# A chunked recurrence beside a matmul chain: TensorE takes the carried part and the state directly behind the scores

## The chip, the cores and the metric

The kernel runs on one core of one Trainium2 chip. The metric is the device time of one execution in microseconds; the figure for the kernel before is the median of three runs.

## The reference

```python
for t in range(S):                                   # batch 4, heads 8, S 768, D 40
    m_new = np.maximum(f_gate[:, :, t] + m, i_gate[:, :, t])
    f_stab = np.exp(f_gate[:, :, t] + m - m_new)
    i_stab = np.exp(i_gate[:, :, t] - m_new)
    C = f_stab * C + i_stab * np.einsum('bhd,bhe->bhde', vt, kt)
    n = f_stab * n + i_stab * kt
    h_tilde = np.einsum('bhde,bhe->bhd', C, qt)
    denom = np.maximum(np.abs(np.einsum('bhd,bhd->bh', n, qt)), 1.0)
    y[:, :, t] = sigmoid(o_gate[:, :, t]) * h_tilde / denom
x = y as [3072, 320]
h = x @ w_in                                         # 320 x 2048
x = (max(h, 0) + alpha * min(h, 0)) @ w_out          # 2048 x 320
h = max(x @ w1, x @ w2, x @ w3)                      # 320 x 768 each
return h @ w_out2                                    # 768 x 320
```

## The kernel before

The recurrence is cut into 24 chunks of 128 tokens (six for each of four batches). Within a chunk all eight heads are done at once: scores (k times q, masked by decays), values (scores times v), the carried part (q times the state at the start of the chunk) and the new state. The layer behind it works on blocks of 2, 3, 3, 4, 4, 4, 4 chunks, so on 256, 384 or 512 columns. For each block it runs 16 "hidden" and 16 "project" steps of 8 matmuls each. While TensorE works on block b, the chunks of block b + 1 are woven in. The last layer runs alone at the end, from about 432 us.

The order of work is one list, `EVERY`, made by `first_plan` and `block_plan`. Each engine runs through the same list and does its own part of each step, waiting on semaphores where it needs another engine. For a chunk the steps are ("scores", ch), ("carry", ch), ("values", ch), ("finish", ...), with "gate" and "pack" for ScalarE and "pack" and "prepare" for GpSimd. A hidden or project step lies between the scores and the carry step. In the blocks of four chunks the order is (H hidden, P project):

```
first chunk:   H0 scores H1 [sigmoid] carry H2 values gate P0 gate finish H3 finish pack prepare P1 pack H4
second chunk:  scores P2 carry H5 P3 values gate ...
third chunk:   P5 scores H8 carry P6 values gate H9 ...
fourth chunk:  H11 scores P9 carry H12 values gate P10 ...
```

The block of chunks 8 to 11 has the same order at 384 columns. Chunks 5, 6 and 7 are spread over a whole block of their own, with more hidden and project steps between them.

What each step does on which engine:
- scores: TensorE does 2 x 4 matmuls (line 653, 16 in the trace), VectorE multiplies each half by the decays (line 1059, tile `prob`) and takes its remainder (line 1063), GpSimd the remainder of that (line 1318).
- carry: TensorE does 3 matmuls for the carried part (line 661) and 3 for the state (line 669), 6 each in the trace. VectorE scales the carried part (line 1073) and makes the new state (lines 1082, 1086).
- values: TensorE does 24 matmuls in bf16 (lines 691, 693, 695), and VectorE sums them (line 1102).
- hidden: ScalarE does a relu of the negated bank (line 913, tile `g_full`), VectorE combines (line 1151), ScalarE rounds it (line 922, tile `g_hi`) and VectorE takes the remainder (line 1132, tile `g_lo`); the last two are done one hidden step later. The project step needs `g_lo`.
- sigmoid (line 828) needs another function table on ScalarE than the exponentials of the gate steps (line 886), so a table is loaded before and after it.

Chunk work on TensorE writes to a ring of three PSUM banks. `TASKS` lists the tasks in the order of `EVERY`: scores0, scores1, carry, state, values0, values1 for a chunk, and one for a turn (transposing a finished chunk). A task takes the bank of the task three before it and waits until that one's reader is done (`drained`): for state this is `prob_done` of scores0, which VectorE signals from line 1059. `UNSPLIT` is 5, the first chunk of the third block; from there on the values are done in three bf16 parts.

Of the kernel before, what the change touches and what calls it, by code (L numbers as in the profile page):

```python
# [62 lines left out]
UNSPLIT = FIRST[2]  # L63
# [115 lines left out]
def high(ap):  # L179

    return ap.bitcast(BF16)[(slice(None),) * (len(ap.shape) - 1) + (slice(1, None, 2),)]
# [7 lines left out]
def build(nc, f_g, i_g, q_t, k_t, kv, o_g, w_in, w_out, alpha, w_max, w_out2, out):  # L189
    with ExitStack() as ctx:  # L190
# [371 lines left out]
        def _(pe):  # L562
# [5 lines left out]
            def turns(n):  # L568

                if n == 0:  # L570
                    pe.wait_ge(gates_done, 1)
                    pe.wait_ge(ident_set, 1)
                    span, table_rows, at = SPANS[0], (V,), 0
                if n == 1:
                    pe.wait_ge(exps_done, 1)
                    pe.wait_ge(tables_set, 1)
                    span, table_rows, at = SPANS[0], (E, W), PLAIN * B * H
                if n == 2:
                    pe.wait_ge(exps_done, 2)
                    pe.wait_ge(gated, 1)  # L580
                    span, table_rows, at = SPANS[1], (V, E, W), 0
                for row in table_rows:
                    for c in range(*span):
                        ins = pe.transpose(turned_at[n][:, at:at + B * H], gates[0:B * H, row, c * L:(c + 1) * L],
                                           ident[0:B * H, 0:B * H])
                        at += B * H
                ins.then_inc(turned, 1)

            def bcast(ch):

                if ch == 0:
                    pe.wait_ge(pick_set, 1)
                    pe.wait_ge(later_set, 2)
                    pe.wait_ge(gates_done, 1)
                if ch == 2:
                    pe.wait_ge(gates_done, 2)
                    pe.wait_ge(gated, 3)
                t = slice(ch * L, (ch + 1) * L)
                for g in range(NG):
                    ps = spread[ch][g]  # L600
                    for k in range(HG):
                        pe.matmul(ps[:, k * L:(k + 1) * L], ident_b[:, :], later[:, :], start=(k == 0), stop=False,
                                  skip_group_check=True)
                    for k in range(HG):
                        ins = pe.matmul(ps[:, k * L:(k + 1) * L], pick[:, g * HG + k, :], gates[:, U, t],
                                        start=False, stop=True, skip_group_check=True)
                    ins.then_inc(spread_out, 1)

            def decays():

                pe.wait_ge(last_set, 1)
                pe.wait_ge(tables_set, 3)
                pe.matmul(acc[0][:, 256:256 + NCH * H], last[:, :], tables[:, 1, :, :].rearrange("p c h -> p (c h)"),
                          start=True, stop=True).then_inc(decays_out, 1)
# [14 lines left out]
            def task(part, ch):  # L629

                n = TASKS.index((part, ch))
                if n >= RING_BANKS:
                    pe.wait_ge(*drained(n - RING_BANKS))
                return ring[n % RING_BANKS]

            def attention(step):
                kind, ch = step[0], step[-1]
                if kind == "decays":
                    return decays()
                ch = step[1]  # L640
                if kind == "turns":
                    turns(ch)
                if kind == "bcast":
                    bcast(ch)
                c = ch % SLOTS
                nth = ch // SLOTS + 1
                if kind == "products" or (kind == "scores" and ch >= PLAIN):
                    pe.wait_ge(qk_loaded[c], QK_LOADS * nth)
                    for g in range(NG):
                        ps = task(f"scores{g}", ch)  # L650
                        for k in range(HG):
                            h = g * HG + k
                            ins = pe.matmul(ps[:, k * L:(k + 1) * L], kt[0:KR, c, h % KH * NK + h // KH, :], qt[0:KR, c, h // KH, :],  # L653
                                            start=True, stop=True)
                        ins.then_inc(scored, 1)
                if kind == "carry" and ch:
                    ps = task("carry", ch)
                    pe.wait_ge(state_ready, ch + 1)
                    for g in range(NK):
                        o = g * KH * DE  # L660
                        ins = pe.matmul(ps[:, g * COLS:(g + 1) * COLS], qt[0:KR, c, g, :], state[0:KR, o:o + COLS],  # L661
                                        start=True, stop=True)
                    ins.then_inc(carry_out, 1)
                if (kind == "carry" and ch != 1) or kind == "late":
                    ps = task("state", ch)
                    pe.wait_ge(v_weighted, ch + 1)
                    for g in range(NK):
                        o = g * KH * DE
                        ins = pe.matmul(ps[0:KR, g * COLS:(g + 1) * COLS], nat[:, c, g * KR:(g + 1) * KR],  # L669
                                        v_w[:, c, o:o + COLS], start=True, stop=True)  # L670
                    ins.then_inc(state_out, 1)
                if kind == "values":
                    if ch < UNSPLIT:
                        pe.wait_ge(nat_loaded[c], 16 * nth)
                    else:
                        pe.wait_ge(v_packed, ch - UNSPLIT + 1)
                    for g in range(NG):
                        ps = task(f"values{g}", ch)
                        if ch < UNSPLIT:
                            pe.wait_ge(prob_done, NG * ch + g + 1)  # L680
                            for k in range(HG):
                                h = g * HG + k
                                v = VO + h * DE
                                ins = pe.matmul(ps[:, k * 3 * DE:k * 3 * DE + DE], prob[:, h, :], nat[:, c, v:v + DE],
                                                start=True, stop=True)
                        else:
                            pe.wait_ge(prob_split, NG * (ch - UNSPLIT) + g + 1)
                            for k in range(HG):
                                h, o = g * HG + k, k * 3 * DE
                                v = v_parts[:, h, :, :].rearrange("p n d -> p (n d)")  # L690
                                pe.matmul(ps[:, o:o + 3 * DE], high(prob[:, h, :]), v, start=(k == 0), stop=False,  # L691
                                          skip_group_check=True)
                                pe.matmul(ps[:, o:o + 2 * DE], high(prob_r[:, h, :]), v[:, 0:2 * DE], start=False,
                                          stop=False, skip_group_check=True)
                                ins = pe.matmul(ps[:, o:o + DE], prob_3[:, h, :], v[:, 0:DE], start=False,
                                                stop=True, skip_group_check=True)
                        ins.then_inc(values_out, 1)
                if kind == "turn":
                    ps = task("turn", ch)
                    pe.wait_ge(y_ready, ch + 1)  # L700
                    at = ch - FIRST[BLOCK_OF[ch]]
                    for a in range(3):
                        ins = pe.transpose(ps[:, a * 128:(a + 1) * 128], y[:, at, Y_AT[a]:Y_AT[a] + 128], ident[:, :])
                    ins.then_inc(turned_out, 1)
# [48 lines left out]
            for s in EVERY:  # L753
                layer1(s) if s[0] in LAYER1 else attention(s)
# [624 lines left out]
```

## Time and profile before

| | us |
|---|---|
| median of three runs | 756.58 (755.68 to 757.09) |
| the profiled execution | 756.52 |
| its span | 754.8 |
| TensorE busy in it | 744.0 (99%) |
| VectorE, ScalarE, GpSimd busy | 465.2, 307.1, 184.9 |

The profile is of one execution. PE is TensorE, PEld its weight loads, DVE VectorE, ACT ScalarE, POOL GpSimd, SP SyncE. A line of the timeline has the start of a run of like instructions, the time that it covers, engine, line, operation and tiles; in brackets stands how long the engine had been idle before it and what ended that. Matmuls are pipelined, so each lasts longer than its distance to the next one; distances between starts tell the throughput.

### The profile page before, as it was taken

The page shows a single profiled execution, that of the slowest core. Times are in us where ns is not written, and L with a number is a line of the kernel's source. Part 1 is how long each engine was busy: PE and PEld are TensorE (multiplying, and loading weights), DVE is VectorE, ACT ScalarE, POOL GpSimd, SP SyncE. Part 2 cuts the span into 40 slices and gives each one's busy share as a digit, 9 for nine tenths or more (in the row PEclk, how much of TensorE's full clock was granted, in tenths as well). Part 3 has the DMA queues.
Part 4 walks back from the last instruction along what each step waited for, and adds up shares of the span by engine and source line. Part 5 has one row for each costly group of instructions (what it writes and reads, how often), then busy time and mean ns, then how long its engine had stood idle before and what let it go on. Part 6 is the DMA issues. An engine that isn't in the chain of part 4 may idle for free.

```text
span 754.8 us, 11652 instructions
## 1 busy us (share of the span) xinstructions
PE 744.0 (99%) x4472; PEld 658.5 (87%) x4472; DVE 465.2 (62%) x792; ACT 307.1 (41%) x646; POOL 184.9 (25%) x213
## 2 busy tenths in 40 slices
PE   9889999999999999999999999999999999999998
PEld 6889999999988888888888888888888888888887
DVE  8877788789788758875887646724342423324232
ACT  6655654653564446435643347221212112121211
POOL 6794334355244324432442000000000000000000
PEclk9999999999999999999999999999999999999999
DMA  9963232232232214221300090030201002010100
GB/s 233 289 194 114 79 105 67 85 108 67 80 111 83 75 41 135 70 82 46 101 1 1 21 296 1 0 119 1 78 0 44 34 1 76 1 36 0 36 1 35
DMA packets 30407, 55.66 MB, mean 74 GB/s; under 512 B 3176, under 2 KB 19024, under 8 KB 29968
## 3 DMA queue, kind: packets, MB, share of 16 engines
q1 hardware_dynamic: 29888, 54.49, 23.6%
q8 instruction: 35, 0.57, 0.3%
q10 hardware_dynamic: 464, 0.43, 0.2%
q14 instruction: 20, 0.16, 0.1%
HBM read 46.96 MB, written 7.95 MB: 73 GB/s over the span
## 4 chain that ended last, share of the span: by engine, by line
PE 87%; DVE 3%; POOL 3%; issue 2%; DMA 2%; SPq 1%; ACT 0%; POOLq 0%; DVEq 0%; ACTq 0%
PE bank L767 26%; PE bank L730 21%; PE bank L745 5%; PE bank L747 5%; PE bank L746 5%; PE bank L653 4%; PE bank L782 3%; PE bank L784 3%; PE bank L783 3%; PE bank L749 3%; PE bank L750 3%; PE bank L669 2%; PE bank L661 2%; DMA u_bcast<-u_scratch 2%; PE bank L691 1%
## 5 line engine op out<-in xcount | busy, mean ns | idle before, releaser
L730 PE MATMUL bank<-x_split,w_hi 128*128 128x512 f32 (+2 forms) x560 | 168.2, 368 | 0.0
L730 PE MATMUL bank<-x_split,w_lo 128*128 128x512 f32 (+2 forms) x336 | 120.9, 362 | 0.0
L913 ACT ACTIVATE g_full<-bank 128x512 f32<-128x512 f32 (+2 forms) x112 | 59.8, 534 | 140.6 <-PE bank L730 139.6
L730 PEld LDWEIGHTS bank<-x_split,w_hi 128*128 128x128 f32 x560 | 103.3, 190 | 12.3 <-ACT x_split L871 0.3
L1151 DVE SCALAR_TENSOR_TENSOR g_full<-g_full,beta,bank 128x512 f32<-128x512 f32 (+2 forms) x112 | 74.7, 667 | 40.4 <-ACT g_full L913 39.8
L1132 DVE TENSOR_TENSOR g_lo<-g_full,g_hi 128x512 fp32r<-128x512 f32 (+2 forms) x112 | 77.8, 694 | 28.6 <-ACT g_hi L922 27.9
L1172 DVE TENSOR_TENSOR best<-bank,first_of_max 128x512 f32<-128x512 f32 x36 | 24.9, 692 | 102.4 <-PE bank L767 76.1
L745 PE MATMUL bank<-g_hi,wproj 128*128 128x512 f32 (+2 forms) x224 | 84.5, 377 | 3.2 <-DVE g_lo L1132 3.2
L922 ACT ACTIVATE g_hi<-g_full 128x512 fp32r<-128x512 f32 (+2 forms) x112 | 63.1, 563 | 51.1 <-DVE g_full L1151 50.9
L747 PE MATMUL bank<-g_hi,wproj 128*128 128x512 f32 (+2 forms) x224 | 80.9, 361 | 0.0
L746 PE MATMUL bank<-g_lo,wproj 128*128 128x512 f32 (+2 forms) x224 | 80.6, 360 | 0.0
L954 ACT ACTIVATE g_hi<-best 128x512 fp32r<-128x512 f32 x36 | 22.8, 632 | 128.7 <-DVE best L1176 128.7
L767 PE MATMUL bank<-x_split_b,w_hi 128*128 128x512 f32 x270 | 70.4, 391 | 0.0
L767 PE MATMUL bank<-x_split_a,w_hi 128*128 128x512 f32 x270 | 70.4, 391 | 0.0
L730 PEld LDWEIGHTS bank<-x_split,w_lo 128*128 128x128 f32 x336 | 64.2, 191 | 6.8
L1318 POOL TENSOR_TENSOR prob<-prob_rest 128x512 bf16<-128x512 f32 x38 | 42.8, 1126 | 75.2 <-DVE prob_rest L1063 75.2
L767 PEld LDWEIGHTS bank<-x_split_a,w_hi 128*128 128x128 f32 x270 | 50.1, 188 | 9.5
L767 PEld LDWEIGHTS bank<-x_split_b,w_hi 128*128 128x128 f32 x270 | 50.0, 188 | 9.3
L886 ACT ACTIVATE u_bcast<-u_bcast,tables 128x128 f32<-128x128 f32 x168 | 52.4, 390 | 0.1
L1307 POOL TENSOR_TENSOR v_rest<-kv,v_parts 128x320 f32<-128x320 f32 x19 | 15.1, 797 | 140.7 <-ACT v_parts L862 140.7
L745 PEld LDWEIGHTS bank<-g_hi,wproj 128*128 128x128 f32 x224 | 42.5, 190 | 8.1 <-DVE g_lo L1132 3.8
L1176 DVE TENSOR_TENSOR best<-bank,best 128x512 f32<-128x512 f32 x36 | 24.9, 692 | 39.5 <-PE bank L767 39.5
(135 smaller groups left out, 1453.3 us busy)
## 6 DMA issues: line engine op xcount, KB each, us to landing
u_bcast<-u_scratch SPq DMA_DIRECT2D x21, 512.0 KB, 4.2
kv<-in_kv SPq DMA_DIRECT2D x24, 324.0 KB, 3.0
q_t<-in_q_t SPq DMA_DIRECT2D x24, 180.0 KB
k_t<-in_k_t SPq DMA_DIRECT2D x72, 60.0 KB
out<-final SPq DMA_DIRECT2D x5, 640.0 KB, 3.8
wproj_raw<-in_w_out SPq DMA_DIRECT2D x4, 640.0 KB, 10.5
o_gate<-in_o_gate SPq DMA_DIRECT2D x4, 640.0 KB, 4.9
w_raw<-in_w_max SPq DMA_DIRECT2D x2, 1152.0 KB, 6.7
```

The lines of the kernel that those rows point to most:

```text
L653: ins = pe.matmul(ps[:, k * L:(k + 1) * L], kt[0:KR, c, h % KH * NK + h // KH, :], qt[0:KR, c, h // KH, :], start=True, stop=True)
L730: ins = pe.matmul(ps[:, 0:cols], w[:, a, f], xs[:, x, 0:cols], start=(m == 0), stop=(m == 7))
L745: pe.matmul(acc[a][:, 0:cols], wa, hi, start=(j == 0), stop=False)
L746: pe.matmul(acc[a][:, 0:cols], wa, lo, start=False, stop=False)
L747: pe.matmul(acc[a][:, 0:cols], wl, hi, start=False, stop=(j == J1 - 1))
L767: ins = pe.matmul(ps[:, :], w[:, a, cols], x2[b2 % 2][:, x, :], start=(k == 0), stop=(k == 7))
L886: ins = act.activation(ub[:, c, h, :], src, ACT.Exp, bias=tables[:, 0, ch, h:h + 1])
L913: act.activation(gf[:, n % GF_SLOTS, 0:cols], hid[j % HID_BANKS][:, 0:cols], ACT.Relu, scale=-1.0).then_inc(neg_done, 1)
L922: act.activation(gh[:, n % G_SLOTS, 0:cols], gf[:, n % GF_SLOTS, 0:cols], ACT.Copy).then_inc(g_hi_done, 1)
L1132: dve.tensor_tensor(gl[:, n % G_SLOTS, 0:cols], gf[:, n % GF_SLOTS, 0:cols], gh[:, n % G_SLOTS, 0:cols].bitcast(F32), ALU.subtract).then_i ...
L1151: dve.scalar_tensor_tensor(out=g, in0=g, scalar=beta[:, j:j + 1], in1=hid[j % HID_BANKS][:, 0:cols], op0=ALU.mult, op1=ALU.add).then_inc(h ...
L1318: pool.tensor_tensor(prob_3[:, heads, :], prob_r[:, heads, :], high(prob_r[:, heads, :]), ALU.subtract).then_inc(prob_split, 1)
```

## The change

For chunks 5 to 23, TensorE issues the matmuls of the carried part and of the state as part of the scores step, directly behind those of the scores, and nothing in the carry step. The list of tasks, the banks and the order of work on all other engines stay as they are. Chunks 0 to 4 are unchanged.

```diff
-                if kind == "carry" and ch:
+                joined = ch >= UNSPLIT
+                if (kind == "carry" and ch and not joined) or (kind == "scores" and joined):
                     ps = task("carry", ch)
                     pe.wait_ge(state_ready, ch + 1)
                     for g in range(NK):
...
                     ins.then_inc(carry_out, 1)
-                if (kind == "carry" and ch != 1) or kind == "late":
+                if (kind == "carry" and ch != 1 and not joined) or kind == "late" or (kind == "scores" and joined):
                     ps = task("state", ch)
                     pe.wait_ge(v_weighted, ch + 1)
                     for g in range(NK):
```

## Rows read from the trace of the kernel before

**Rows 1.** The page, part 1: busy us, share of the span, instructions.
```profile
PE 744.0 (99%) x4472; PEld 658.5 (87%) x4472; DVE 465.2 (62%) x792; ACT 307.1 (41%) x646; POOL 184.9 (25%) x213
```
**Rows 2.** Waits of TensorE: who waited for whom, us in total, times, longest.
```profile
PE bank L745 <- DVE g_lo L1132: 3.2, 3, 2.5
PE bank L703 <- DVE y L1118: 2.5, 1, 2.5
```
**Rows 3.** Timeline of TensorE, chunk 12.
```profile
205.54 1.95 PE L653 MATMUL bank<-q_t,k_t 120*128 120x128 f32 x16
207.25 0.48 PE L730 MATMUL bank<-x_split,w_hi 128*128 128x512 f32 x1
207.57 0.40 PE L730 MATMUL bank<-x_split,w_lo 128*128 128x512 f32 x1
...
209.17 0.83 PE L661 MATMUL bank<-state,q_t 120*128 120x128 f32 x6
209.84 0.83 PE L669 MATMUL bank<-v_weighted,kv 128*120 128x128 f32 x6
210.42 0.47 PE L730 MATMUL bank<-x_split,w_hi 128*128 128x512 f32 x1
```
**Rows 4.** Timeline of TensorE, the scores of chunks 5, 9, 10 and 13.
```profile
84.25 1.95 PE L653 MATMUL bank<-q_t,k_t 120*128 120x128 f32 x16
...
154.83 1.95 PE L653 MATMUL bank<-q_t,k_t 120*128 120x128 f32 x16
...
168.73 1.95 PE L653 MATMUL bank<-q_t,k_t 120*128 120x128 f32 x16
...
220.68 1.95 PE L653 MATMUL bank<-q_t,k_t 120*128 120x128 f32 x16
```
**Rows 5.** Timeline of VectorE, first product of chunks 5, 9, 10, 12 and 13.
```profile
85.50 0.69 DVE L1059 TENSOR_TENSOR prob<-bank,u_bcast 128x512 f32<-128x512 f32 x1
...
157.46 0.68 DVE L1059 TENSOR_TENSOR prob<-bank,u_bcast 128x512 f32<-128x512 f32 x1
...
170.76 0.68 DVE L1059 TENSOR_TENSOR prob<-bank,u_bcast 128x512 f32<-128x512 f32 x1
...
207.04 0.69 DVE L1059 TENSOR_TENSOR prob<-bank,u_bcast 128x512 f32<-128x512 f32 x1
...
220.61 0.78 DVE L1132 TENSOR_TENSOR g_lo<-g_full,g_hi 128x512 fp32r<-128x512 f32 x1 [0.71 <-ACT g_hi L922]
221.51 0.75 DVE L1151 SCALAR_TENSOR_TENSOR g_full<-g_full,beta,bank 128x512 f32<-128x512 f32 x1
222.18 0.69 DVE L1059 TENSOR_TENSOR prob<-bank,u_bcast 128x512 f32<-128x512 f32 x1
```
**Rows 6.** Timeline of ScalarE, one row ahead of chunk 9, then chunk 12 to 13.
```profile
156.12 0.47 ACT L913 ACTIVATE g_full<-bank 128x384 f32<-128x384 f32 x1
...
209.37 0.60 ACT L913 ACTIVATE g_full<-bank 128x512 f32<-128x512 f32 x1 [1.58 <-PE bank L730]
209.98 1.28 ACT L828 ACT_TABLE_LOAD   x1
...
219.59 0.48 ACT L865 ACTIVATE v_parts<-v_rest 128x320 bf16<-128x320 f32 x1 [0.89 <-POOL v_rest L1307]
...
220.88 0.60 ACT L913 ACTIVATE g_full<-bank 128x512 f32<-128x512 f32 x1 [0.30 <-PE bank L730]
```
**Rows 7.** Waits of all engines: a weight load of the values for the carried part.
```profile
PEld bank L691 <- DVE carried L1073: 0.2, 1, 0.2
```
**Rows 8.** Stretches: length, busy us by engine (instructions), TensorE's granted clock, DMA share, GB/s.
```profile
26.00:29.40 3.40, 0.94 (x9) 0.93 (x9) 2.96 (x8) 3.37 (x7) 0.79 (x2) 1.00 1.08 249
29.40:32.90 3.50, 3.50 (x18) 3.24 (x17) 2.62 (x5) 1.96 (x5) 3.44 (x5) 0.51 1.06 302
39.70:43.10 3.40, 1.39 (x12) 1.18 (x11) 1.32 (x2) 1.23 (x4) 3.40 (x5) 1.00 1.09 269
43.10:46.50 3.40, 2.87 (x13) 2.87 (x14) 3.36 (x8) 2.50 (x8) 2.97 (x5) 0.50 0.97 297
```

## The prediction

> **What bounds the kernel now.** I read the busy times first: TensorE works 744.0 us of a span of 754.8 [rows 1]. Next came the list of waits of its engine. It has five entries, all before the sixth chunk's work; the two largest are in [rows 2]. So in the region of the change (84 to 432 us, blocks 1 to 5) TensorE never idles by the profile. It sets the end, and every new wait there adds to the time unless something that it issues gets shorter. After that I read the timeline around single chunks, engine by engine, to see how late each engine could be without TensorE noticing.
>
> **What is moved.** For 19 chunks (5 to 23) the six matmuls of the carried part (C) and the six of the state (T) come directly behind the 16 of the scores (S), and the hidden or project step that stood between comes after them. Nothing is removed or added; no DMA is moved in its queue. The operands of C and T are ready early: the state vector since the chunk before, the weighted v since two chunks before. The loads of q and k that wait for T can start about 1.5 to 1.9 us sooner; SP had no late load in this region and none of its transfers appears among TensorE's waits, so I cost that at nothing, in both directions.
>
> **What the switches of kind cost.** In chunk 12, S starts at 205.54, the first matmul of the next hidden step at 207.25, its second at 207.57, C at 209.17, T at 209.84, hidden again at 210.42 [rows 3]. A matmul of C or T stands 0.11 us behind the last (0.67/6). The first big matmul behind small ones takes 0.32 us to its successor instead of 0.23. That looks like 0.09 us per return to big matmuls, and the move takes away one return per chunk. But 16 matmuls at 0.1115 should take 1.78 us and S took 1.71: the last small one is followed 0.07 us early. Net, one return costs 0.02 us. Gain: 19 x 0.02 = **-0.4 us**. The other end is the face value, 19 x 0.085 = -1.6 us.
>
> **The new wait.** The PSUM ring has three banks, and tasks take them in turn: scores0, scores1, carry, state. So T writes the bank of scores0 and must wait until VectorE has multiplied it (`prob_done`, line 1059). Before, a big step (1.4 to 1.9 us) lay between; now only scores1 and C do. T's first weight load would go out 21 spacings behind the first of S: 21 x 0.1115 = S + 2.34 us. Behind a waiting T stand the project or hidden steps, so the whole wait is lost. When is VectorE done? I set its first `prob` of a chunk against the start of that chunk's scores:
> - chunk 5: 84.25 against 85.50 + 0.69, ready at S + 1.94 [rows 4, 5]. Chunks 7, 8 and 11 are the same within 0.05, chunk 6 is at 1.78: no wait, 0.35 us or more spare.
> - chunk 12: 205.54 [rows 3] against 207.04 + 0.69: ready at S + 2.18. With some 0.05 for the signal this is 0.1 us ahead of 2.34: no wait, but hardly any cover. Chunks 15, 16, 19, 20, 23 are alike; 14, 18 and 22 are at 1.79.
> - chunk 9: 154.83 against 157.46 + 0.68: S + 3.31, a wait of 1.0 us already by these rows. Chunk 10: 168.73 against 170.76 + 0.68: S + 2.70, a wait of 0.4 us.
> - chunks 13, 17, 21: 220.68 against 222.18 + 0.69: S + 2.18 as well, by the trace of before. But these move.
>
> **What the move itself makes later.** The first chunk of blocks 3 to 5 and chunk 8 have the order hidden0, S, hidden1, C, T, hidden2, values. The move puts hidden1 behind C and T, 12 x 0.1115 = 1.34 us later (the step after it ends where it did before, since only the order inside changed). ScalarE waits for just that step: its relu at 209.37 had been idle 1.58 us for TensorE [rows 6]. Behind that relu stand two table loads of 1.28 us, the sigmoid of a whole block and eight exponentials, back to back, and none of it can start before: no idle entry stands between 209.37 and the 0.89 us at 219.59, and that one is a wait for GpSimd, whose step follows ScalarE's own one before it. Only at 220.88 does ScalarE wait for TensorE again, and only 0.30 us. So the 1.34 us of delay travels the whole way, and at least 1.04 of it arrive at the relu of hidden4.
> - chunk 13: ScalarE's g_hi comes ahead of that relu and ends the full 1.34 later, so VectorE's g_lo, which waited for it, goes from 220.61 to 221.95, and the step behind it to about 222.60, 0.65 us behind (it was at 221.51); the product goes from 222.18 to 223.27 and is done at 223.95, S + 3.27 [rows 5]. With 0.05 for the signal the wait is 3.32 - 2.34 = **0.98 us**. Chunks 17 and 21 have the same rows: 3 x 0.98 = 2.9 us.
> - chunk 9: ScalarE's relu at 156.12 starts with no idle time before it, 1.1 us after its hidden step ended [rows 6], so ScalarE is already the late one and the delay arrives whole: 3.31 + 1.34 = 4.65, wait 4.70 - 2.34 = **2.36 us**.
> - chunk 5 also has this order, but four hidden and project steps more lie before the next scores, and chunk 6's product was waiting for TensorE: covered.
> - chunk 10: its VectorE chain starts anew from a wait for TensorE (behind its hidden6), so it moves with TensorE: wait 2.75 - 2.34 = **0.41 us**. In return the 0.2 us that the values of chunk 10 waited for the carried part [rows 7] go, since VectorE does not move and TensorE comes later: -0.2 us.
> - The third chunks (14, 18, 22 and 10) also have their hidden step moved behind C and T. There VectorE's carried part would end near S + 6.9 and the second half of the values needs it at S + 7.2, and the delay is used up in ScalarE's and VectorE's waits for TensorE before the next scores. In the second and fourth chunks a project step is moved, for which no engine waits.
>
> **The sum.** 2.36 + 0.41 + 2.9 - 0.2 - 0.4 = +5.1 us. The profiled execution took 756.52 us (span 754.8), 0.06 below the median of the runs, so both give the same: **761.6 us**, 0.7% slower.
>
> **The rivals.**
> *The clock falls too.* TensorE was granted its full clock but for two stretches: 29.4 to 32.9 at 0.51 and 43.1 to 46.5 at 0.50, that is the lower of its levels (1.2 instead of 2.4 GHz). Ahead of each it had been busy only 0.94 of 3.40 us and 1.39 of 3.40 us [rows 8], in waits of 2.5 us each [rows 2]. The wait at chunk 9 would be of that size. If the clock falls there for as long, at most half of 3.4 us is lost; I take 1.5: **763.1 us**. Against it: 2.36 is a little shorter, and the matmuls around it are denser. The Trainium skill ("TensorE: Matmul & The Clock Gate", section "Why this matters for your kernels") wants gaps between bursts kept short to avoid throughput drops mid-kernel, and its figure for a harmful gap lies above all waits here; by it there is no fall at chunk 9, while the trace shows one behind each wait of 2.5 us. The measurement decides, so the chance stays with the trace: 0.25.
> *Only block 2 is late.* In the 512-column blocks a step of TensorE is 1.82 us and ScalarE's chain may catch up (GpSimd's part may overlap more than I let it). Then the 2.9 us go: 758.7 us. Against: the back-to-back rows [rows 6]. Chance 0.10.
> *Not slower.* The other side: the delay of ScalarE's chain is absorbed in every block, because the relu of hidden1 is done early enough in slack that I don't see, and only the 1.0 and 0.4 us of chunks 9 and 10 stay. With the returns at face value: 756.5 + 1.4 - 0.2 - 1.6 = 756.1; with my price 757.3. It decides between 0.5 and 1.3 us of slack on ScalarE between the relu of hidden1 and the next scores. The trace has 0.30 in chunk 13, none in chunk 9. Chance 0.13, of which 0.04 for faster.
> *More waits.* The six chunks with 0.1 us of cover miss it, or GpSimd and VectorE slow each other as they meet anew (the remainder at 1063 took 0.69 to 1.5 us in different chunks). Six times 0.3 on top: 763.4 us. Chance 0.10.
>
> **How the numbers follow.** Forecast 0.42, clock 0.25, block 2 alone 0.10, not slower 0.13, more waits 0.10. The range 757.5 to 764.5 leaves out the not-slower case and the joint case of clock and more waits. A measurement can tell about 0.2% (1.5 us) from no change. Slower by more than that (over 758.1): 0.85; within: 0.11; faster: 0.04.
>
> **What would show it.** TensorE's list of waits gets line 669 for VectorE's line 1059: about 2.4 us at chunk 9, 1.0 at chunks 13, 17, 21, 0.4 at chunk 10. If 13, 17 and 21 are missing, the chain through ScalarE was judged wrong; if the small ones (12, 15, 16 ...) appear, the cover of 0.1 us. A granted clock of 0.5 behind chunk 9 shows the clock rival. ScalarE's relu of the step behind C and T should start 1.3 us later against S. The forecast is wrong if T isn't held at all, or if TensorE's small matmuls run closer than 0.11 us when 28 of them stand together.

## The result and the profile after

| | before | after |
|---|---|---|
| median, us | 756.59 (755.68 to 757.09, 4 runs) | 762.75 (761.66 to 763.40, 4 runs) |
| ratio | | 1.0083, 95% interval 1.0067 to 1.0099 |
| profiled execution, its span, us | 756.52, 754.8 | 761.66, 759.9 |

The kernel got 0.8% slower, 6.2 us by the medians. 761.6 had been forecast, in a range of 757.5 to 764.5.

The two profiled executions differ by less (5.1 us). The part ahead of the change varies: the scores of chunk 5, with the same code ahead of them, started at 84.25 us before and at 82.77 us here, and at 83.1 to 85.3 us in the profiles of the experiments below. That 761.66 meets the forecast of 761.6 almost to the digit is therefore luck: the medians stand 1.1 us higher, and so do the terms, as the stretch shows. I therefore compare the traces over one stretch, from the start of the first matmul of the scores of chunk 5 to the start of the last matmul of all. The two ends in the trace of after (timeline of TensorE):

```profile
82.77 1.95 PE L653 MATMUL bank<-q_t,k_t 120*128 120x128 f32 x16
...
756.58 0.31 PE L785 MATMUL bank<-wout_hi,g_lo 128*128 128x320 f32 x1
```
and the last matmul in the trace of before, whose first end is in [rows 4]:
```profile
751.47 0.31 PE L784 MATMUL bank<-wout_hi,g_lo 128*128 128x320 f32 x1
```
That is 673.81 against 667.22 us: **+6.59 us** in the stretch.

TensorE's waits in the changed kernel (engine, tile and line, waited for whom: us in total, times, longest; line 670 is line 669 of before, 1060 is 1059):
```profile
PE bank L670 <- DVE prob L1060: 4.4, 4, 2.1
PE bank L704 <- DVE y L1119: 2.5, 1, 2.5
PE bank L746 <- DVE g_lo L1133: 2.2, 2, 1.7
...
PEld bank L670 <- DVE prob L1060: 5.5, 5, 2.3
```
The first line has taken the top over [rows 2]: the state's matmuls wait for the product that frees the bank of scores0. TensorE as a whole sees four such waits, its weight loads five; the fifth is chunk 10's, of 0.3 us. Below, S + x means x us behind the start of that chunk's scores, and C and T stand for the carried part (line 662) and the state (line 670). Here are chunk 9, with the longest, then chunks 12 (none) and 13, on TensorE:
```profile
153.21 1.95 PE L653 MATMUL bank<-q_t,k_t 120*128 120x128 f32 x16
155.00 0.83 PE L662 MATMUL bank<-state,q_t 120*128 120x128 f32 x6
157.96 1.63 PE L670 MATMUL bank<-v_weighted,kv 128*120 128x128 f32 x6 [2.13 <-DVE prob L1060]
159.25 0.67 PE L746 MATMUL bank<-g_hi,wproj 128*128 128x384 f32 x1
159.71 0.52 PE L747 MATMUL bank<-g_lo,wproj 128*128 128x384 f32 x1
...
207.87 1.95 PE L653 MATMUL bank<-q_t,k_t 120*128 120x128 f32 x16
209.65 0.83 PE L662 MATMUL bank<-state,q_t 120*128 120x128 f32 x6
210.32 0.82 PE L670 MATMUL bank<-v_weighted,kv 128*120 128x128 f32 x6
210.90 0.47 PE L731 MATMUL bank<-x_split,w_hi 128*128 128x512 f32 x1
...
222.98 1.95 PE L653 MATMUL bank<-q_t,k_t 120*128 120x128 f32 x16
224.76 0.83 PE L662 MATMUL bank<-state,q_t 120*128 120x128 f32 x6
226.36 0.92 PE L670 MATMUL bank<-v_weighted,kv 128*120 128x128 f32 x6 [0.76 <-DVE prob L1060]
227.03 0.47 PE L746 MATMUL bank<-g_hi,wproj 128*128 128x512 f32 x1
```
From C to T is 0.67 us where nothing waits (chunk 12). In chunk 13 it is 1.60, so 0.93 us were waited, and T then takes 0.67 instead of 0.58 us to what follows: a wait costs 0.1 us more to start again. In chunk 9 it is 2.96 us: a wait of 2.29 us.

Where the lateness of chunk 13 comes from shows on ScalarE; these lines answer to [rows 6]:
```profile
213.02 0.60 ACT L914 ACTIVATE g_full<-bank 128x512 f32<-128x512 f32 x1 [2.92 <-PE bank L731]
213.64 1.28 ACT L829 ACT_TABLE_LOAD   x1
214.93 1.27 ACT L829 ACTIVATE o_gate<-o_gate 128x1280 f32<-128x1280 f32 x1
...
217.23 1.28 ACT L887 ACT_TABLE_LOAD   x1
218.52 2.45 ACT L887 ACTIVATE u_bcast<-u_bcast,tables 128x128 f32<-128x128 f32 x8
...
223.24 0.48 ACT L866 ACTIVATE v_parts<-v_rest 128x320 bf16<-128x320 f32 x1 [0.89 <-POOL v_rest L1308]
223.61 0.61 ACT L923 ACTIVATE g_hi<-g_full 128x512 fp32r<-128x512 f32 x1
224.13 0.58 ACT L914 ACTIVATE g_full<-bank 128x512 f32<-128x512 f32 x1
```
The first relu now waits 2.92 instead of 1.58 us, 1.34 us more; its hidden step starts 3.03 instead of 1.71 us behind the scores, 1.32 later. Against the scores of chunk 12 it starts at 5.15 instead of 3.83. The last relu no longer waits for TensorE at all: ScalarE has become the late one. On VectorE this gives, ahead of chunk 13 (answering to [rows 5]):
```profile
224.26 0.78 DVE L1133 TENSOR_TENSOR g_lo<-g_full,g_hi 128x512 fp32r<-128x512 f32 x1 [0.71 <-ACT g_hi L923]
224.97 0.73 DVE L1152 SCALAR_TENSOR_TENSOR g_full<-g_full,beta,bank 128x512 f32<-128x512 f32 x1
225.62 0.68 DVE L1060 TENSOR_TENSOR prob<-bank,u_bcast 128x512 f32<-128x512 f32 x1
```
The product is done at 226.30, 3.32 us behind the start of the scores (before: 2.18).

Then there is the clock. The stretches around the wait of chunk 9 (length, busy us by engine, granted clock, DMA; they answer to [rows 8]):
```profile
154.50:157.80 3.30, 1.33 (x12) 1.14 (x11) 2.70 (x5) 1.72 (x4) 3.30 (x4) 1.00 0.00 0
157.80:161.20 3.40, 3.24 (x12) 3.24 (x13) 3.33 (x6) 0.06 (x1) 2.77 (x4) 0.50 0.13 38
```
TensorE was busy 1.33 of 3.30 us, and then was granted 0.50 of its clock, the level of 1.2 GHz, for 3.4 us. Before, the clock was full here. T at chunk 9 took 1.29 us instead of 0.67 to what follows it, and the project step 2.37 instead of 1.48: 1.5 us together.

The +6.59 us of the stretch thus fall into: waits with restart 2.39 (chunk 9), 0.39 (chunk 10), 3 x 1.02 (13, 17, 21) = 5.84; the lower clock 1.5; less 0.23 for the values of chunk 10, which no longer wait for the carried part [rows 7]; less about 0.5 for 19 returns to big matmuls. That makes 6.6.

### The profile page after: what moved, and what is told of

It reads as the page before. It is cut to its first block, busy times and chain, and to the rows that moved or that the text cites. A ratio compares the mean times of both kernels' runs of the same rounds, so it can differ in the third digit from the quotient of the medians.

```text
span 759.9 us, 11652 instructions
## 1 busy us (share of the span) xinstructions
PE 745.5 (98%) x4472; PEld 659.7 (87%) x4472; DVE 466.2 (61%) x792; ACT 306.3 (40%) x646; POOL 185.4 (24%) x213
## 4 chain that ended last, share of the span: by engine, by line
PE 80%; issue 7%; DVE 5%; POOL 3%; ACT 1%; ACTq 0%; POOLq 0%; DVEq 0%
PE bank L768 26%; PE bank L731 18%; PE bank L746 5%; PE bank L748 5%; PE bank L747 5%; PE bank L783 3%; PE bank L785 3%; PE bank L784 3%; PE bank L653 3%; PE bank L750 2%; PE bank L751 2%; PE bank L670 2%; DVE prob L1060 1%; PE bank L662 1%; PE bank L692 1%
```

## The experiments

Each has a median with the ratio to the kernel before on the same chip, and the time of the stretch (chunk 5's scores to the last matmul) in its profiled execution, where before took 667.22 and the changed kernel 673.81 us. Each stretch is that of a single execution; the changed kernel's, taken twice, came out 0.13 us apart. All start from the changed kernel.

**Only the carried part is moved.**
```diff
-                if (kind == "carry" and ch != 1 and not joined) or kind == "late" or (kind == "scores" and joined):
+                if (kind == "carry" and ch != 1) or kind == "late":
```


> Only the carried part is moved behind the scores; the state stays where it was before. If the loss is the state's wait for the bank of scores0, there is none here, since a whole step lies again before the state: 756.6 us, same as before, though the first product of chunk 13 should still come later than before, by about half of what it does in the changed kernel (S + 2.6 to 2.8 instead of S + 3.3), for the hidden step is put off by 0.67 us. If the loss comes from putting off the hidden steps as such (ScalarE and VectorE late for their own work, the wait only a sign of it), half of the loss stays: 759 to 760 us.

756.57 us, ratio 1.0008 (0.9999 to 1.0016); stretch 667.47. The loss is gone with the state's early place, while the product of chunk 13 was later than before by a little under half of what it is in the changed kernel (S + 2.63, against 2.19 before and 3.32). One small thing I had not expected: chunk 9's product came at S + 4.00, so late that even a state behind the project step was held for 0.2 us, and 0.1 more to start again. So putting the hidden steps off by 0.67 us costs nothing where nobody waits; the whole delay of 1.34 us is in the next run and in that of chunks 8, 12, 16 and 20 alone.

**The five late chunks are left out.**
```diff
-                joined = ch >= UNSPLIT
+                joined = ch >= UNSPLIT and ch not in (9, 10, 13, 17, 21)
```


> The change for 14 chunks; chunks 9, 10, 13, 17 and 21 keep the order of before. My theory: all of the loss sits in the state's wait of these five, so no wait of line 669's matmuls is left, and 756.6 - 14 x 0.02 = 756.3 us. If the small covers of 0.1 us (chunks 12, 15, 16, 19, 20, 23) fail or the moved hidden steps hurt elsewhere: 757.5 to 760 us.

756.96 us, ratio 1.0012 (1.0003 to 1.0020); stretch 667.90. Half a miss. Chunks 10, 13, 17, 21 and the six with 0.1 us of cover did not wait, but chunk 9 did, in the order of before:
```profile
154.46 1.95 PE L653 MATMUL bank<-q_t,k_t 120*128 120x128 f32 x16
...
157.66 0.83 PE L662 MATMUL bank<-state,q_t 120*128 120x128 f32 x6
159.21 0.92 PE L670 MATMUL bank<-v_weighted,kv 128*120 128x128 f32 x6 [0.71 <-DVE prob L1060]
```
Chunk 8 still put off its hidden step, so the product of chunk 9 stood at S + 4.69, and the state reached its place at S + 3.87: I had taken the project step for enough cover without setting it against 4.7. At 13, 17 and 21 the products were as late as in the changed kernel (S + 3.32), and nobody waited. The rest checks the price of a return. The stretch grew by 0.68 us: 0.97 for this wait and its restart, and 0.08 that the values of chunk 9 now waited for the carried part, less 14 returns. So one return is 0.026 us.

**The first chunks are left out.**
```diff
-                joined = ch >= UNSPLIT
+                joined = ch >= UNSPLIT and ch not in (8, 12, 16, 20)
```


> The change for all but the first chunks of the blocks (8, 12, 16 and 20 keep the order of before). My theory: the lateness at chunks 13, 17, 21 and 1.3 us of that at chunk 9 come from the hidden step put off one chunk earlier. So chunks 13, 17, 21 do not wait, chunk 9 waits 1.0 us and chunk 10 0.4 us, each 0.1 more to start again: 756.6 + 1.1 + 0.5 - 0.2 - 0.3 = 757.7 us. Rival: the second chunks are late by themselves, because TensorE takes the state too early there: all five waits stay, 761.5 to 762.5 us.

756.86 us, ratio 1.0011 (1.0002 to 1.0020); stretch 668.01. In the trace it is what my theory said: no wait at 13, 17 and 21, 0.90 us at chunk 9 and 0.30 at chunk 10 and 0.1 more each.
```profile
154.96 1.95 PE L653 MATMUL bank<-q_t,k_t 120*128 120x128 f32 x16
156.74 0.83 PE L662 MATMUL bank<-state,q_t 120*128 120x128 f32 x6
158.31 0.92 PE L670 MATMUL bank<-v_weighted,kv 128*120 128x128 f32 x6 [0.74 <-DVE prob L1060]
```
So the second chunks are not late by themselves; leaving four *other* chunks alone took their waits away. The stretch grew by 0.79 (expected: 1.1), since I had counted the waits at chunks 9 and 10 0.1 us too long each and the returns 0.1 too low together; the median grew by 0.5.

**The sigmoid goes to the end of an earlier block.**
```diff
-        if n == 1 and b:
-            both.append(("sigmoid", b + 1))
...
+    if b + 2 < NBLK:
+        both.append(("sigmoid", b + 2))
     return both + [("rows_out", b)]
```


> The whole change, and the sigmoid of a block is done at the end of the block two before it, behind its last turn, where ScalarE was idle for 2.2 to 3.5 us, instead of behind hidden1. Chunk 8 and the first chunks keep the moved hidden step. My theory: what carries the delay is ScalarE's unbroken chain of two table loads, sigmoid and exponentials; without 3.8 us of it ScalarE waits for TensorE again before the next scores, chunks 9, 13, 17 and 21 do not wait, chunk 10 still waits 0.5 us: 756.6 + 0.5 - 0.2 - 0.4 = 756.5 us. Rival: the delay reaches the next scores by VectorE's own queue whatever ScalarE does: 761 to 762.5 us.

756.88 us, ratio 1.0011 (1.0002 to 1.0020); stretch 667.50. The whole change is in, and the hidden step is put off as in the changed kernel, but there was no wait at chunks 13, 17 and 21. ScalarE and VectorE ahead of chunk 13:
```profile
211.00 0.60 ACT L914 ACTIVATE g_full<-bank 128x512 f32<-128x512 f32 x1 [2.91 <-PE bank L731]
...
221.16 0.60 ACT L914 ACTIVATE g_full<-bank 128x512 f32<-128x512 f32 x1 [0.61 <-PE bank L731]
```
```profile
221.79 0.75 DVE L1152 SCALAR_TENSOR_TENSOR g_full<-g_full,beta,bank 128x512 f32<-128x512 f32 x1 [0.42 <-ACT g_full L914]
222.46 0.68 DVE L1060 TENSOR_TENSOR prob<-bank,u_bcast 128x512 f32<-128x512 f32 x1
```
The first relu is put off as in the changed kernel (2.91 us idle), but the last one waits for TensorE again. What carried the delay was ScalarE's chain. The move took less out of it than the 3.8 us that I had expected: one table load of 1.28 us and the sigmoid of 1.27 are gone, but a load still stands ahead of the exponentials, which start 3.85 us behind the first relu (at 214.85) instead of 5.50. That is 1.65 us less, and it accounts for the wait of the last relu: 0.30 before [rows 6], + 1.65 - 1.34 = 0.61, as measured. Chunk 9 was a partial miss: the product came at S + 2.91, a wait of 0.51 us. There ScalarE's last relu (at 155.35) still didn't wait for TensorE, so even the shorter chain is not caught up in time.

No run has the early sigmoid without the rest. But the terms above (0.61 and 0.40 for the waits at 9 and 10 with their restarts, less 0.23 for the values of chunk 10 and 0.49 for 19 returns) give +0.29 us against +0.28 measured, which leaves next to nothing for the move of the sigmoid itself.

**The parts of the change by chunks.** The changed kernel once more, then chunks 12 to 23 alone, 5 to 11 alone, and 8, 12, 16, 20 alone:
```diff
-                joined = ch >= UNSPLIT
+                joined = ch >= 12
```
```diff
-                joined = ch >= UNSPLIT
+                joined = UNSPLIT <= ch < 12
```
```diff
-                joined = ch >= UNSPLIT
+                joined = ch in (8, 12, 16, 20)
```


> The changed kernel once more, for its clock. Its waits at chunks 9, 10, 13, 17 and 21 must come back at 2.3, 0.3, 0.9, 0.9 and 0.9 us. Theory of the clock: a wait of TensorE of 2.3 us brings the lower clock behind it, as at chunk 9 in the first profile; then the profile shows it again, and from the scores of chunk 5 to the last matmul it takes 673.8 us. Rival: the fall there was chance (how the wait lay in time), and a profile without it takes 672.3 us for the same stretch. Median of the runs 762 to 763 us.

> The change for chunks 12 to 23 alone: waits of 0.9 us at 13, 17 and 21 (0.1 more each to start again) and 12 returns less at 0.025 us, no wait in chunks 5 to 11, no fall of the clock there. If the parts add up: 756.5 + 3.05 - 0.3 = 759.2 us, and 2.75 us more than before from the scores of chunk 5 to the last matmul. If the 512-column blocks take some of the wait back: under 758.5 us.

> The change for chunks 5 to 11 alone. Waits at chunks 9 and 10 (2.4 and 0.4 us with starting again), less 0.2 us for the values of chunk 10 and 7 returns at 0.025 us: +2.4 us from the scores of chunk 5 to the last matmul, and +3.9 us where the clock falls behind chunk 9. So 758.9 us without the fall, 760.4 with it.

> The change for chunks 8, 12, 16 and 20 alone, that is only those that put off a hidden step ahead of ScalarE's long chain. The first product of chunks 9, 13, 17 and 21 is as late as in the changed kernel (S + 4.7 and S + 3.3), but their state comes a project step later: only chunk 9 waits, 0.9 + 0.1 us. 756.5 + 1.0 - 0.1 = 757.4 us. Rival: if the delay itself costs, whoever waits for it, near half of the loss is here: 759 us or more.

| | median, us | ratio to before | stretch, against before |
|---|---|---|---|
| the whole change | 762.49 | 1.0088 (1.0076 to 1.0101) | 673.94, +6.72 |
| chunks 12 to 23 | 758.29 | 1.0034 (1.0023 to 1.0046) | 670.02, +2.80 |
| chunks 5 to 11 | 760.11 | 1.0054 (1.0041 to 1.0067) | 671.11, +3.89 |
| chunks 8, 12, 16, 20 | 757.20 | 1.0017 (1.0008 to 1.0026) | 668.20, +0.98 |

The parts add up: 2.80 + 3.89 = 6.69 against 6.59 and 6.72. For 12 to 23 the waits were the expected 0.93 us three times. The median rose by 2.1 us rather than 2.75 and so fell under the 758.5 that I had named for a wait partly taken back. The trace doesn't bear that out: the three waits are whole and the stretch grew by 2.80. The difference is no larger than the part ahead of chunk 5 varies, and 2.75 us lies within the interval of the ratio. For 5 to 11 stretch and median came as expected with the fall of the clock (+3.9, 760.4). The last kernel has the products of chunks 13, 17 and 21 at S + 3.3, as late as in the changed one, and no wait there, only 0.89 us at chunk 9. Again the delay costs nothing where nobody waits for it.

The clock was low behind the wait at chunk 9 in each of the three profiles that have the wait of 2.3 us with nothing in it. Here the two new ones, the whole change and then chunks 5 to 11:
```profile
157.70:161.00 3.30, 1.18 (x10) 0.99 (x10) 2.66 (x5) 1.72 (x4) 3.30 (x4) 1.00 0.00 0
161.00:164.40 3.40, 3.40 (x14) 3.40 (x13) 3.33 (x6) 0.00 (x0) 2.77 (x3) 0.51 0.30 94
```
```profile
155.50:158.90 3.40, 1.42 (x13) 1.23 (x11) 2.80 (x5) 1.74 (x4) 3.40 (x4) 1.00 0.00 0
158.90:162.30 3.40, 3.26 (x12) 3.26 (x13) 3.33 (x6) 0.04 (x1) 2.77 (x4) 0.50 0.15 33
```
In the profiles with 0.9 us of wait at chunk 9, or at 13, 17 and 21, it stayed full. The granted clock of all the runs agrees: its mean over a run was 0.991 to 0.996 in all 14 runs with that wait, but 0.997 or 0.998 in 25 of the 66 runs of the kernel before that were made with the experiments. One fall of 3.4 us is worth 0.002 of that mean.

**The wait is filled.**
```diff
                     ins.then_inc(carry_out, 1)
+                    if ch == 9:
+                        pe.wait_ge(hid_read, 2 * J1 + 5 - HID_BANKS + 1)
+                        for n in range(10):
+                            pe.matmul(hid[1][:, 0:3 * L], w1h[:, 0, 640:768], xs[:, 0, 0:3 * L], start=True, stop=True)
```


> The whole change, and at chunk 9 TensorE does ten useless matmuls of 384 columns between the carried part and the state; they write to the bank that the next hidden step starts afresh. They take 10 x 0.17 = 1.7 us of a wait of 2.3 us, so the state comes no later. Theory: behind the wait at chunk 9 the clock is halved for 3.4 us and that costs 1.5 us by itself; with TensorE busy in the wait there is no fall, and from the scores of chunk 5 to the last matmul it takes 673.8 - 1.5 = 672.3 us, the median is 1.5 us below that of the changed kernel: 761.0 us. Rival: the lower clock costs nothing that the wait doesn't cost already: 762.5 us as before.

761.31 us, ratio 1.0062 (1.0049 to 1.0075); stretch 672.42, 1.4 to 1.5 us less than the two profiles of the changed kernel. TensorE at chunk 9 (lines 668, 674 and 1064 are the filling, the state and the product here), and the stretches around:
```profile
155.95 0.83 PE L662 MATMUL bank<-state,q_t 120*128 120x128 f32 x6
156.54 2.01 PE L668 MATMUL bank<-x_split,w_hi 128*128 128x384 f32 x10
158.91 0.92 PE L674 MATMUL bank<-v_weighted,kv 128*120 128x128 f32 x6 [0.35 <-DVE prob L1064]
```
```profile
154.00:157.40 3.40, 3.40 (x29) 3.40 (x29) 2.26 (x4) 2.43 (x7) 2.15 (x3) 1.00 0.00 0
157.40:160.80 3.40, 3.05 (x20) 2.73 (x19) 3.33 (x6) 0.52 (x1) 3.40 (x4) 1.00 0.00 0
```
The state starts 2.96 us behind the carried part as without the filling, so the product's lateness is untouched; what is gone is the low clock. It cost 1.5 us on its own. With more work the kernel took less time (ratio to before 1.0062 instead of 1.0088; the two intervals don't meet), and the clock's mean was 0.998 in four of its six runs.

**Both: the sigmoid early, and chunks 9 and 10 left out.** The edit is that of the sigmoid above and `joined = ch >= UNSPLIT and ch not in (9, 10)`.

> The sigmoid at the end of an earlier block, and the change for all chunks but 9 and 10, the only two whose state still waited there. No wait for the bank of scores0 is left, 17 returns less at 0.025 us: 0.4 us below the kernel before from the scores of chunk 5 to the last matmul (666.8 us against 667.2), so 756.0 us and no difference that five rounds can tell. If moving the sigmoid costs at the block's end (rows copied later): 757 us.

755.98 us, ratio 0.9995 (0.9986 to 1.0004); stretch 666.78, no wait of the state left. 17 returns less gave 0.44 us in the stretch, 0.026 us each if the early sigmoid costs nothing; as a time it is no difference.

## Why the prediction was right

The sum's terms against what the runs showed, in us:

| term | forecast | measured |
|---|---|---|
| wait at chunk 9 (product done at S + 4.65) | 2.36 | 2.29 (S + 4.69), and 0.1 to start again |
| wait at chunk 10 | 0.41 | 0.29, and 0.1 |
| waits at 13, 17, 21 (S + 3.27) | 0.98 each | 0.93 each (S + 3.32), and 0.1 |
| chunks with 0.1 us of cover | none | none |
| values of chunk 10 | -0.2 | -0.23 |
| 19 returns | -0.4 | -0.5 (0.026 each) |
| starting again after five waits | none | +0.5, as above |
| the clock behind chunk 9 | none (a rival with 1.5) | 1.5, in three profiles of three |
| the stretch | +5.1 | +6.59 and +6.72 |

- *The mechanism* held: the state waits for the bank of scores0, and two causes make it wait. At chunks 9 and 10 VectorE was already late. At 13, 17, 21, and for 1.3 us more at 9, the delay is made a chunk earlier, by putting hidden1 behind C and T, and ScalarE carries it. Taking away either end of that relay (the first chunks' move, or the sigmoid with one of its two table loads) took the waits away at 13, 17 and 21.
- *The sum* is 1.5 us short, all of it the clock. The other errors cancel: 0.5 us for starting again has no term, while the five waits were together counted 0.34 us too long and the gains (values and returns) 0.13 us too small. That the rest fits so well is in part luck.
- *Return to big matmuls:* netting the long first spacing against the short last one was right. At its face value of 0.085 us, 19 returns would have paid 1.6; the two runs that tell it best, with the five late chunks left out and with both remedies, give 0.026 each.
- *The clock* is the step that failed, as a matter of likelihood. I called 2.36 us "a little shorter" than the waits that had brought the clock down and gave the fall 0.25; it came each time, and the likeliest case should have been 763.1, not 761.6. In the prediction's own terms: the chance of the clock rival was set too low. The medians of 762.75 and 762.49 lie 1.1 and 0.9 above the forecast. The trace of before pointed that way: busy 0.94 and 1.39 of 3.40 us ahead of its two falls [rows 8], and the wait at chunk 9 leaves 1.2 to 1.4. It would not have made the fall certain. Ahead of chunk 5 the twelve profiles have 16 waits of 2.2 us or more, and 14 had a fall around or behind them. The other two, of 2.45 and 2.48 us, had none: with the five late chunks left out and with the sigmoid early, TensorE was busy 0.95 and 0.92 of the 3.40 us up to 30.0, and the clock stayed full up to 36.0. And the length of the wait alone doesn't decide: of two waits at the same place, one of 1.51 us (the last run) was followed by a fall and one of 1.48 (chunks 12 to 23) was not. What else decides is open. The Trainium skill ("TensorE: Matmul & The Clock Gate", section "Why this matters for your kernels") wants no gaps over about 3 us and would have let waits of this size pass; these traces don't agree.
- *Only block 2 is late* fell with chunks 12 to 23 alone (+2.80 us). *Not slower* fell too: ScalarE's slack was 0.30 us in chunk 13 as read. *More waits*: the six chunks at S + 2.18 stayed without a wait in every kernel.
- One reading was wrong without a consequence: of TensorE's five waits in the kernel before, four lie ahead of chunk 5, but the fifth (0.4 us, line 782) stands at 749.76 in the last layer, behind the region of the change.
- What stays open is why the part ahead of chunk 5 varies by some 2 us from run to run with the same code. It is larger than several effects here; no run was made for it. The traces show where it sits: TensorE's wait for `g_lo` that ends near 43 us (line 746) lasted 1.70 us in the first profile of the changed kernel and 3.62 in the second, which reached chunk 5 at 82.77 and 85.30. And it goes with the clock: of the 66 runs of the kernel before, the 14 with a mean granted clock of 0.993, the lowest among them, took 757.2 us on average, the others 756.0.

## What to carry to other kernels

When a step is moved up on the engine that is the bound, look at both of its neighbours. It may reach a buffer that is not free yet, and what it pushes back may start a chain on another engine that has no slack until much later; set the first engine's need and the last one's delivery against the same start, chunk by chunk. A step that leaves the order of the bound engine denser by kind may save only what first and last spacing leave when taken together. And a new wait of over 2 us on TensorE should be priced with the clock behind it, as the likelier case: 17 of the 19 in these profiles had a fall around or behind them.

## What was not expected of the hardware

- A single wait of 2.3 us of TensorE, in a region where it had no other gap of over 1 us, was followed by 3.4 us at 0.50 of its clock in three profiles of three; ten useless matmuls in the wait gave back the 1.5 us. Elsewhere in the kernel two waits of 2.45 and 2.48 us passed at the full clock. Waits of 0.9 us, fifteen in the profiles here, brought none.
- After each wait on a semaphore, at the full clock, the state's six matmuls took 0.67 to 0.68 us to what follows instead of 0.58.
